# Reordering the steps around the first MLPs of an attention + two-MLP kernel, and choosing other weight blocks to split ahead

## The reference

```python
# attention: batch 4, heads 8, seq 576, head_dim 64, fp32
scores = 0.125 * np.matmul(q, k.transpose(0, 1, 3, 2))
kth = np.partition(scores, -32, axis=-1)[..., -32:-31]      # the 32nd largest of a row
scores = np.where(scores >= kth, scores, -1e9)
attn = softmax(scores)                                       # sum + 1e-9
x = np.matmul(attn, v)        # to (2304 tokens, 512)
# first MLP, d_ff 1536
x = (sigmoid(x @ w_gate) * (x @ w_val)) @ w_out
# second MLP, d_ff 2048
x = np.maximum(x @ w_in, 0.0) ** 2 @ w_out2
```

## Time and profile before

| what | value |
|---|---|
| median of 3 runs | 1176.14 us (1176.04 to 1177.05) |
| the profiled execution's own time | 1176.16 us |
| its span, first to last instruction | 1174.3 us |
| PE busy | 1132.5 us (96%) |
| DVE, ACT, POOL busy | 838.3, 676.4, 623.5 us |
| DMA | 270.13 MB, 68.5% of 16 engines |

### The profile page before, as it was taken

The page is one execution under the profiler, slowest core; times in us unless marked ns, Lnnn a source line. Parts: engine busy times, 40 slices in busy tenths (PEclk is TensorE's granted clock), DMA queues, the critical chain, the costliest instruction groups (busy, mean ns, idle before and its releaser), DMA issues.

```text
span 1174.3 us, 21809 instructions
## 1 busy us (share of the span) xinstructions
PE 1132.5 (96%) x7520; PEld 998.2 (85%) x7520; DVE 838.3 (71%) x1756; ACT 676.4 (58%) x1758; POOL 623.5 (53%) x539
## 2 busy tenths in 40 slices
PE   4579999999999999999999999999999999999999
PEld 2459989999989999999888787888888888899998
DVE  7999998788997898999777688975666683011130
ACT  5886777776875765776565557755544464112130
POOL 4987687776885555675445436643443365012130
PEclk7789999999999999999999999999999999999999
DMA  9988877988888666767655555665455555577784
GB/s 356 349 307 286 281 264 246 311 274 290 274 281 310 217 213 222 217 226 234 207 164 174 178 177 192 211 197 187 172 165 172 172 163 172 192 250 250 257 252 139
DMA packets 90397, 270.13 MB, mean 230 GB/s; under 512 B 10032, under 2 KB 16176, under 8 KB 90288
## 3 DMA queue, kind: packets, MB, share of 16 engines
q1 hardware_dynamic: 90288, 268.74, 68.5%
HBM read 228.33 MB, written 40.37 MB: 229 GB/s over the span
## 4 chain that ended last, share of the span: by engine, by line
PE 88%; DVE 7%; issue 2%; ACT 1%; SPq 1%; POOL 1%; DMA 1%; ACTq 0%; POOLq 0%
PE ps L648 21%; PE ps L650 21%; PE ps L649 21%; PE ps L634 7%; PE ps L589 7%; PE ps L549 6%; PE ps L565 5%; DVE work L850 3%; DVE top L848 3%; DMA heads_in<-qk_in 1%; SPq L470 1%; DVE g_lo L885 1%; POOL below L917 0%; POOL full_buf L957 0%; POOL probs L922 0%
## 5 line engine op out<-in xcount | busy, mean ns | idle before, releaser
L848 DVE MAX8 top<-work 128x8 f32<-128x576 f32 x432 | 312.3, 751 | 0.5
L917 POOL TENSOR_TENSOR below<-scores,below 128x576 f32<-128x576 f32 x120 | 174.2, 1451 | 237.8 <-ACT below L700 237.6
L648 PE MATMUL ps<-xy_hi,ring 128*128 128x512 f32 (+2 forms) x800 | 286.4, 358 | 0.0
L650 PE MATMUL ps<-xy_hi,ring 128*128 128x512 f32 (+2 forms) x800 | 281.4, 352 | 0.0
L649 PE MATMUL ps<-xy_lo,ring 128*128 128x512 f32 (+2 forms) x800 | 281.1, 351 | 0.0
L850 DVE MATCH_REPLACE8 work<-top,work 128x576 f32<-128x576 f32 x288 | 214.1, 743 | 0.0
L648 PE MATMUL ps<-g_hi,ring 128*128 128x384 f32 (+2 forms) x560 | 200.4, 358 | 0.3 <-DVE g_lo L885 0.3
L650 PE MATMUL ps<-g_hi,ring 128*128 128x384 f32 (+2 forms) x560 | 196.9, 352 | 0.0
L649 PE MATMUL ps<-g_lo,ring 128*128 128x384 f32 (+2 forms) x560 | 196.8, 351 | 0.0
L648 PEld LDWEIGHTS ps<-xy_hi,ring 128*128 128x128 f32 x800 | 150.2, 188 | 18.5 <-issue 6.9
L650 PEld LDWEIGHTS ps<-xy_hi,ring 128*128 128x128 f32 x800 | 150.1, 188 | 12.9
(11 more groups left out here) (70 smaller groups left out, 1709.8 us busy)
## 6 DMA issues: line engine op xcount, KB each, us to landing
ring<-w_split SPq DMA_DIRECT2D x318, 512.0 KB, 4.2
wring<-w_in SPq DMA_DIRECT2D x113, 256.0 KB, 5.3
w_split<-stage SPq DMA_DIRECT2D x46, 512.0 KB, 4.7
w_split<-ring SPq DMA_DIRECT2D x22, 512.0 KB, 6.0
vt<-v_in SPq DMA_DIRECT2D x16, 480.0 KB, 6.0
heads_in<-qk_in SPq DMA_DIRECT2D x16, 336.0 KB, 4.6
vt<-v_in SPq DMA_DIRECT2D x16, 320.0 KB, 3.2
heads_in<-qk_in SPq DMA_DIRECT2D x16, 304.0 KB, 4.4
```

The costliest lines, as they stand in the source:

```text
L648: nc.tensor.matmul(dst, w_hi, hi[:, k, 0:WIDTH[c]], start=first, stop=False)
L650: mm = nc.tensor.matmul(dst, w_lo, hi[:, k, 0:WIDTH[c]], start=False, stop=final)
L848: nc.vector.max(out=best, in_=sc if step == 0 else wk).then_inc(sel_step[t % 2], 1)
L917: nc.gpsimd.tensor_tensor(out=below[:, t % 2, :], in0=scores_of(t), in1=below[:, t % 2, :], op=ALU.subtract).then_inc(mask_done, 1)
```

## The change

- **Which blocks are split ahead.** Blocks 0 to 15 instead of every third one: 16 splits ahead instead of 23. They stay in SBUF (STAY), so that chunk 0 doesn't load them again, and their 16 loads fall away. From block 16 on, even blocks are split during chunk 0 (26 of them, where 23 were, and none among its first 16 blocks) and odd blocks during chunk 1 (26 instead of 22). Loads of plain blocks go from 113 to 94, loads of split ones from 318 to 314. The splits ahead are spread over slots 1 to 11.
- **Tile 11** (LAST_ALONE, the last tile of chunk 0). In slot 12 DVE does steps 0 and 1 of tile 12, then steps 4, 5, 6 of tile 11 in a row. ACT does find_below and enlarge of tile 11 at the end of slot 12, POOL its mask ahead of tile 10's normalise, ACT its exp ahead of unit 6's copy_pt.
- **ACT before the first MLPs** splits weights at the start of a slot.
- **DVE's order.** Up to slot 93: evac of the first and the second list come together, after steps 4, 0, 5, 1, and ahead of steps 6, 2, 3. In chunk 0's tiles invert comes after step 3 instead of before it. From slot 94 another order: 0, 4, evac, 5, 1, 6, evac, 2, 3, evac.
- **ACT and POOL** put split_x later, and from slot 94 find_below first on ACT and mask after the first evac on POOL.
- **The lists.** The second list gets a third of a slot's halves rounded down; in a DOUBLE slot the first list has at least 2 and the second none (BETWEEN). From slot 94 PE does the first scores between the first and the second list.

```diff
-JOBS = [(None, n, True, True) for n in range(0, NB, CLASSES)]
+WHEN = [0 if n < 16 else (1, 2)[n % 2] for n in range(NB)]
+
+STAY = 16
+JOBS = [(None, n, True, True) for n in [*range(STAY, NB), *range(STAY)] if WHEN[n] == 0]
 NPRE = len(JOBS)
-JOBS += [(c, n, c + 1 == n % CLASSES, c < NW or c == NW and n % CLASSES == CLASSES - 1)
+JOBS += [(c, n, c + 1 == WHEN[n], c < NW or c == NW and WHEN[n] == CLASSES - 1)
          for c in range(NC) for n in range(NB)]
 NWHOLE = NPRE + NW * NB
+STAYS = [k for k in range(NPRE, NPRE + STAY) if k >= WPLACES and JOBS[k - WPLACES][:2] == (None, JOBS[k][1])]
...
+LAST_ALONE = CHUNK_END[0]
...
-BETWEEN = 0
+BETWEEN = 2
...
-            b = (len(todo) + 1) // 3
+            b = len(todo) // 3
...
+AHEAD_SPLITS = 4
 for _k in range(NPRE):
-    SPLIT_AT.setdefault(1 + _k * (MLP_AT[0] - 2) // NPRE, []).append(_k)
+    SPLIT_AT.setdefault(1 + _k * (MLP_AT[0] - AHEAD_SPLITS) // NPRE, []).append(_k)
...
             def load_weights(k):
+                if k in STAYS:
+                    return
...
             for s in range(min(SCORE_AT) + 1, MLP_AT[0]):
-                if 0 <= s - MASK:
+                for k in SPLIT_AT.get(s, []):
+                    split_weights(k)
+                if 0 <= s - MASK and s - 2 != LAST_ALONE:
                     find_below(s - MASK)
                     enlarge(s - MASK)
-                for k in SPLIT_AT.get(s, []):
-                    split_weights(k)
...
+                if s - 1 == LAST_ALONE:
+                    find_below(LAST_ALONE)
+                    enlarge(LAST_ALONE)
...
-            for s in range(SLOTS):
-                if s in NORM_AT and s >= MLP_AT[0]:
+            for s in range(MLP_AT[3]):
+                if s in NORM_AT and UNITS[TILES[NORM_AT[s]][0]][0] >= LATE:
                     invert(NORM_AT[s])
                 for c, n in blocks_of(SHARES[s - 1][2]) if s else []:
                     evac(c, n)
-                select_both(s, [0])
-                select_both(s, [1])
+                select_if(s - 1, 4)
+                select_if(s, 0)
+                select_if(s - 1, 5)
+                select_if(s, 1)
                 for c, n in blocks_of(SHARES[s][0]):
                     evac(c, n)
-                select_both(s, [2])
-                if s in NORM_AT and s < MLP_AT[0]:
+                for c, n in blocks_of(SHARES[s][1]):
+                    evac(c, n)
+                if s - 1 == LAST_ALONE:
+                    for step in range(4, 7):
+                        select(s - 1, step)
+                select_if(s - 1, 6)
+                select_if(s, 2)
+                if s - 2 == LAST_ALONE:
+                    invert(LAST_ALONE)
+                select_if(s, 3)
+                if s in NORM_AT and UNITS[TILES[NORM_AT[s]][0]][0] < LATE and s - 2 != LAST_ALONE:
                     invert(NORM_AT[s])
...
-            for s in range(SLOTS):
-                if 0 <= s - MASK < NT:
+            for s in range(MLP_AT[3]):
+                if 0 <= s - MASK < NT and s - MASK != LAST_ALONE:
                     mask(s - MASK)
                 for c, n in blocks_of(SHARES[s - 1][2]) if s else []:
                     evac(c, n)
-                for c, n in blocks_of(SHARES[s][0]):
-                    evac(c, n)
                 for k in SPLIT_AT.get(s - 1, []):
                     split_weights(k)
+                for c, n in blocks_of(SHARES[s][0]):
+                    evac(c, n)
+                if s - 1 == LAST_ALONE:
+                    mask(LAST_ALONE)
                 if s in NORM_AT:
                     normalise(NORM_AT[s])
```

More of the change, by code:

```diff
@@ L422, in wait_loaded @@
             if k < NWHOLE:
-                eng.wait_ge(whole_loaded[k % WPLACES], 16 * (k // WPLACES + 1))
+                loads = sum(i % WPLACES == k % WPLACES and i not in STAYS for i in range(k + 1))
+                eng.wait_ge(whole_loaded[k % WPLACES], 16 * loads)
             else:
@@ L658, in _ @@
                         score(t)
-            for s in range(SLOTS):
+            for s in range(MLP_AT[0]):
+                for u in SCORE_AT.get(s, []):
+                    for t in tiles_of(u):
+                        score(t)
+                for u in PROD_AT.get(s, []) if s < MLP_AT[0] - 1 else []:
+                    times_v(u)
+                for u in PROD_AT.get(s, []) if s == MLP_AT[0] - 1 else []:
+                    times_v(u)
+                if s in TURN_AT:
+                    turn(TURN_AT[s])
+            for s in range(MLP_AT[0], MLP_AT[3]):
                 for c, h in SHARES[s][0]:
@@ L666, in _ @@
                         score(t)
+                for u in PROD_AT.get(s, []):
+                    times_v(u)
+                for u in SCORE_AT.get(s, [])[1:]:
+                    for t in tiles_of(u):
+                        score(t)
+                for c, h in SHARES[s][2]:
+                    mlp_half(c, h)
+                if s in TURN_AT:
+                    turn(TURN_AT[s])
+            for s in range(MLP_AT[3], SLOTS):
+                for c, h in SHARES[s][0]:
+                    mlp_half(c, h)
+                for u in SCORE_AT.get(s, [])[:1]:
+                    for t in tiles_of(u):
+                        score(t)
+                for c, h in SHARES[s][1]:
+                    mlp_half(c, h)
                 for u in PROD_AT.get(s, []):
@@ L798, in _ @@
                     copy_x(u)
-                last = s == MLP_AT[0] - 1
-                if last:
+                if s == MLP_AT[0] - 1:
                     copy_pt(TURN_AT[s - 1])
-                if 0 <= s - MASK:
+                if s - 2 == LAST_ALONE:
+                    exp(LAST_ALONE)
+                if 0 <= s - MASK and s - 2 != LAST_ALONE:
                     exp(s - MASK)
@@ L808, in _ @@
                         copy_x(u)
-            for s in range(MLP_AT[0], SLOTS):
+            for s in range(MLP_AT[0], MLP_AT[3]):
                 for u in SCORE_AT.get(s - 1, [])[-1:]:
@@ L824, in _ @@
                         copy_scores(t)
-                for c, p in X_AT.get(s, []):
-                    split_x(c, p)
                 if s - MASK < NT:
@@ L830, in _ @@
                     evac(c, n)
+                for c, p in X_AT.get(s, []):
+                    split_x(c, p)
                 for u in PROD_AT.get(s, []):
                     copy_x(u)
+            for s in range(MLP_AT[3], SLOTS):
+                if s - MASK < NT:
+                    find_below(s - MASK)
+                    enlarge(s - MASK)
+                for u in SCORE_AT.get(s - 1, [])[-1:]:
+                    for t in tiles_of(u):
+                        copy_scores(t)
+                for c, n in blocks_of(SHARES[s - 1][2]):
+                    evac(c, n)
+                if s - 1 in TURN_AT:
+                    copy_pt(TURN_AT[s - 1])
+                for c, n in blocks_of(SHARES[s][0]):
+                    evac(c, n)
+                for u in SCORE_AT.get(s, [])[:-1]:
+                    for t in tiles_of(u):
+                        copy_scores(t)
+                if s - MASK < NT:
+                    exp(s - MASK)
+                for u in PROD_AT.get(s, []):
+                    copy_x(u)
+                for c, p in X_AT.get(s, []):
+                    split_x(c, p)
+                for c, n in blocks_of(SHARES[s][1]):
+                    evac(c, n)
             for c, n in blocks_of(SHARES[SLOTS - 1][2]) + blocks_of(REST):
@@ L851, in select, with select_if @@
                                             imm_value=-3.0e38).then_inc(sel_step[t % 2], 1)
-            def select_both(s, steps):
-                for step in steps:
-                    if 0 <= s - 1 < NT and step < 3:
-                        select(s - 1, 4 + step)
-                    if s < NT:
-                        select(s, step)
+            def select_if(t, step):
+                if 0 <= t < NT and (t != LAST_ALONE or step < 4):
+                    select(t, step)
             def invert(t):
@@ L979, in _ @@
                     evac(c, n)
+            for s in range(MLP_AT[3], SLOTS):
+                for c, n in blocks_of(SHARES[s - 1][2]) if s else []:
+                    evac(c, n)
+                for k in SPLIT_AT.get(s - 1, []):
+                    split_weights(k)
+                if 0 <= s - MASK < NT and s - MASK != LAST_ALONE:
+                    mask(s - MASK)
+                if s in NORM_AT:
+                    normalise(NORM_AT[s])
+                for c, n in blocks_of(SHARES[s][0]):
+                    evac(c, n)
+                for c, n in blocks_of(SHARES[s][1]):
+                    evac(c, n)
+                for c, p in X_AT.get(s, []):
+                    split_x(c, p)
             for c, n in blocks_of(SHARES[SLOTS - 1][2]) + blocks_of(REST):
```

31 lines of the change are left out of this document (26 added, 5 removed).

## The result

The changed kernel takes 1183.92 us (median of 6 runs, 1183.35 to 1188.04), where the kernel before takes 1176.29 beside it: 1.0069 times as long, 95% interval 1.0055 to 1.0083. It is 7.6 us slower, outside the range 1172.8 to 1180.2. Its profiled execution took 1183.87 us, 1182.1 of it span.

A forecast was written before the change was run, and what follows sets the result against it. PE was taken to bound the kernel, with DVE setting the pace up to 80 us. Start -0.5, chunk 0 +1.6, chunk 1 -0.8 and the wait at 528 -0.1 gave +0.2: 1176.3 us, range 1172.8 to 1180.2.

The forecast's parts named there:

- Later slots only change order; PE is full there, turns lie far behind their normalise: Slots after chunk 1's wait at 333.12: no cost, 0 us, with ends -0.3 and +1.
- the same for the small wait at 528: -0.1: PE's small wait at 528 us: an earlier g_lo from DVE's new evac order saves 0.1 us.
- slower by POOL: Rival: three added h-block splits cost PE 3.8 us, and chunk 1's stretch g_lo by 1.09 each; 1180.9 us, chance 0.18.
- Chunk 1: PE's 1.57 us wait at 333.12 shrinks through an earlier g_lo: -0.8 us, ends -1.57 and +0.6.
- block 55's split: Chunk 1, on ACT: now stands in front of the evac that PE's wait hangs on, costing 0.6 us.
- Chunk 0: H blocks at 145 to 177 us: more splits on POOL delay turns, +1.6 us, ends 0 and 3.8.
- The term for unit 15: Near 157 us: mask 26 and tile 25's normalise come 1.1 us late, and with no slack the turn too, +1.1 us.
- The start: Up to the first MLP blocks: later MLP start against a removed PE wait near 86 us, net -0.5 us.
- The delay of unit 6's turn: Near 72.31 us: tile 11's mask ahead of tile 10's normalise makes the turn 1.15 us later.
- The 1.22 us at 86.5: PE's wait for val 0's evac in slot 15 goes, since DVE reads it after four steps instead of seven.
- Loads: DMA: 6.75 MB less, mostly before 80 us, and denser stores from block 16, cost PE 0 us.
- Doesn't do what it says: Rival: tile 11 isn't ahead where it counts; already in the sum as +0.1 to +1.1 us, no separate chance.

The follow-up runs named there:

- undo_both: Changed kernel with both DVE's order of evacs (to slot 93) and the lists put back as before; its total isn't given, chunk 2 measured -0.51 us.
- thirds: Kernel before with the new blocks split ahead and kept, but from block 16 two of three split in chunk 0, every third in chunk 1; 1187.51 us.
- undo_order: Changed kernel with DVE's evac of the second list back behind steps 6 and 2, slots 15 to 93; five runs between 1180.0 and 1183.7 us.
- only_blocks: Kernel before with the new choice of blocks to split, and their loads' waits, and nothing else; 1180.38 us.
- tile11_undone: Changed kernel with tile 11 treated as any other tile of chunk 0 on all engines; 1183.17 us.
- one_list: Changed kernel, but in slot 85 alone the second list takes two halves; its total isn't given, PE's wait in chunk 2 was 3.08 us.

## Why the prediction was wrong

**The step that failed** is "Later slots only change order; PE is full there, turns lie far behind their normalise", priced at 0, with "the same for the small wait at 528: -0.1". Measured: +5.70 us in chunk 2. I asked there only whether turns wait for POOL. I didn't ask which engine has no idle time beside PE. The windows above, of the kernel before, answer it: DVE 52.90 of 53.00 us. The wait of 0.26 us at 528.59 named DVE's g_lo and was the sign that DVE had no reserve; I read it as a gain to be had. I also had the price: the earlier trace rows show a g_lo stretched by 1.09 us. I tied it to the added splits alone, though the mask reads SBUF too and stands in every slot, and lists that move blocks to the slot's start move their g_lo's beside it. What the runs showed in place of the 0: in chunk 2 the g_lo's grew from 12.27 to 14.84 us, PE waited 3.42 us for one and lost 1.7 more to the clock, and with masks that read nothing the loss was gone (-0.39). For the rival "slower by POOL" I had put 1180.9; its price was of the right kind, though it counted one stretched g_lo where it named two or three; its place (splits, chunk 1) was not right.

**Chunk 1**, -0.8, has the wrong sign: +1.28 (of which the wait at 335.02 is 2.56 instead of 1.57). The gain from the earlier g_lo isn't there. undo_both, with DVE's old order, loses 1.16, hardly less than after. What I priced at 0.6 as the counterweight, block 55's split, was one of a denser row of splits, and these delay the square for which ACT waits. thirds shows that the number of splits in chunk 1 is the cause.

**Chunk 0**, +1.6, cost +0.32 in after and +0.80 with the choice of blocks alone. The mechanism is partly there: the wait near 157 for POOL is 0.21 us where 1.1 was foretold, and there is one of 0.47 us at 187.29 for unit 18, 0.5 foretold. The second names ACT's copy of the scores, which stands behind an exp that waited 1.77 us for POOL's mask. The term for unit 15 was too large: the mask of tile 26 comes at 152.78 instead of 152.67, 0.11 us later and not 1.1, since the mask before it starts at 145.97 instead of 146.84. thirds bounds the other side, with 5.94 us up to unit 20 (1.7 of it clock) for three more h splits and their like.

**The start**, -0.5, was +0.05. DVE's wait near 25 us is gone in this execution:

```profile
24.89 0.16 DVE L929 RECIPROCAL rinv<-rsum_eps 128x1 f32<-128x1 f32 x1
```

That it always goes isn't shown: the eight other kernels with this invert behind step 3 wait there between 0.25 and 1.37 us, the four without it between 0.91 and 2.27. The delay of unit 6's turn held, foretold as 1.15 and found as 1.15 (-0.28 at unit 4, +0.87 at unit 6). The sum erred in letting the clock give back half of it. Turn 6 took 2.18 us, no less than before, so the delay passes to the MLPs undiminished, and 0.67 us were added between turn 6 and the first matmul of the MLPs, 0.62 of it where a stretch at 1.2 GHz now lay over scores and products (scores 2.29 us instead of 1.94, products 1.58 instead of 1.31). The first MLP matmul at 81.37 lies outside the 79.9 to 80.9 that I had named. The 1.22 us at 86.5 went, as foretold, but partly by luck: undo_order shows that a start so late loses that wait with the old order too. 1.54 us late and 1.49 regained make the +0.05.

**Loads**, 0, held: no PE wait names a ring, and the bytes are 263.06 MB for 263.4 foretold; the 6.75 was in units of 1024 x 1024 bytes, 7.08 MB, which gives 263.05. **Doesn't do what it says** was nearer than I thought: tile 11's unit is ready earlier, and PE comes to it later.

After minus before, term by term, on the profiled execution: start +0.05 (up to unit 8, with the -0.28 ahead of unit 4), chunk 0 +0.32, up to unit 28 another +0.25, chunk 1 +1.28, chunk 2 +5.70, later +0.16, in all +7.76.

## What to carry to other kernels

Before pricing a reordering at nothing because the bound engine is full, look in each stage for the second engine without idle time; a small wait that names it is a warning, not a gain. A list or order that moves work in time also moves what it runs beside. Here that lengthened DVE's two-input subtractions from 12.27 to 14.84 us in the one stage where DVE had no time to spare, while over the whole kernel they stayed as long as they were. When the last tile ahead of a stage is moved up, find the work from which the waiting engine runs through; only what comes before that moves the stage.

## What the runs showed of the hardware

**The clock behind a wait.** PE's waits of 1.57 us near 333 (before, thirds) were never followed by a lower clock in the traces. Those of 2.46 to 2.58 us near 335 were four times without it (after, undo_both, only_blocks, tile11_undone), once with 3.4 us at 1.2 GHz (one_list) and in four kernels with 6.8 us. The longer ones, 3.08 to 3.42 us in chunk 2, had 3.4 us behind them each time, and thirds shows 3.4 us behind a wait of 2.17 and 6.8 us around one of 2.95. Where 6.8 us came, they cost more than the wait itself: between units 28 and 30 undo_order lost 4.17 us and after 1.28, with waits of 2.48 and 2.56. The window of undo_order:

```profile
335.50:342.30 6.80, 6.38 (x48) 5.19 (x50) 6.70 (x16) 4.05 (x12) 5.09 (x6) 0.50 0.58 209
```

Its five runs fall into 1180.0 and 1180.3 on one side and 1182.7 to 1183.7 on the other, a gap of about that size. Why the same wait draws it in one execution and not in another stays open, and so a difference of up to 3 us between two of these kernels' profiled executions says nothing by itself; the stage columns say something when they are read with the clock column.

**A subtraction beside a mask.** g_lo (128 x 384, both inputs in SBUF) took 0.55 us alone and 1.46 to 1.71 when it began within 0.4 us behind the start of POOL's mask, and 1.52 beside POOL's xy_lo. It then ended 0.41 us behind POOL's operation. The other way round POOL is held: a mask that began 0.2 us behind the start of a g_lo took 1.75 us, and 1.43 to 1.44 where no g_lo was running at its start. A memset on POOL, which reads nothing, left a pair of g_lo's at 1.01 us.
